# A linear-attention scan with two dense blocks on one NeuronCore: tokens taken apart by parity, the jobs of a slot in another order, and the last level's scores copied by ScalarE

## What is computed

```
for t in range(S):
    cur = einsum('bhd,bhe->bhde', u[None] * k[t], v[t])
    y[t] = einsum('bhd,bhde->bhe', r[t], state + cur)
    state = w[t][:, :, :, None] * state + einsum('bhd,bhe->bhde', k[t], v[t])
```

```
h = gelu(x @ w_in); u, v = split(h)
gated = u * (einsum('ts,bsd->btd', w_sg, layernorm(v) * g_ln) + b_sg)
x = x + gated @ w_out
xk, xr = mu * x + (1 - mu) * x_prev          # one mix for k, one for r
out = sigmoid(xr @ w_r) * ((relu(xk @ w_k) ** 2) @ w_v)
```

## Time and profile before

| | us |
|---|---|
| median of three runs | 417.6 |
| the profiled execution | 420.01 |
| its span, first to last instruction | 418.3 |
| TensorE matmuls busy | 364.8 (87%) |
| VectorE busy | 253.9 (61%) |
| ScalarE busy | 190.4 (46%) |
| GpSimd busy | 120.9 (29%) |

### The profile page before, as it was taken

How to read it: one execution, slowest core, us unless ns; L and a number is a source line. 1 busy time by engine, 2 the same in 40 slices (tenths; PEclk the granted TensorE clock), 3 DMA queues, 4 the chain that set the end, 5 groups by cost and what they waited for, 6 DMA issues and landing times.

```text
span 418.3 us, 9108 instructions
## 1 busy us (share of the span) xinstructions
PE 364.8 (87%) x3836; PEld 344.8 (82%) x3836; DVE 253.9 (61%) x384; ACT 190.4 (46%) x326; POOL 120.9 (29%) x138
## 2 busy tenths in 40 slices
PE   5665868978878698668999999999999999999997
PEld 4554657767768586568998999999999999999996
DVE  6357867687979967650655445998796311764011
ACT  4435626666774645533312416627783700565100
POOL 6705524346447343000000000610970000463000
PEclk9998958989999999969999999999999999999999
DMA  8986670606202110101000001306000011000011
GB/s 161 233 199 134 177 175 3 133 15 141 60 4 60 30 30 2 30 2 49 19 2 0 0 2 26 126 0 196 15 2 0 2 40 55 19 2 0 19 39 56
DMA packets 58584, 23.59 MB, mean 56 GB/s; under 512 B 52656, under 2 KB 56112, under 8 KB 58544
## 3 DMA queue, kind: packets, MB, share of 16 engines
q1 hardware_dynamic: 58544, 23.02, 21.8%
HBM read 18.29 MB, written 2.36 MB: 49 GB/s over the span
## 4 chain that ended last, share of the span: by engine, by line
PE 78%; issue 7%; ACT 7%; DVE 6%; DVEq 0%; ACTq 0%
PE ps L1184 20%; PE ps L1186 19%; PE ps L1185 19%; PE ps L1175 5%; PE ps L1107 5%; PE ps L1171 3%; PE ps L1140 2%; PE ps L1129 2%; ACT r L617 1%; DVE kT L860 1%; PE ps L1117 1%; ACT rU L615 1%; PE ps L1145 1%; ACT ktok L639 1%; ACT yT L672 1%
## 5 line engine op out<-in xcount | busy, mean ns | idle before, releaser
L552 POOL TENSOR_TENSOR r<-r,wb 112x768 f32<-112x768 f32 x24 | 41.3, 1732 | 83.9 <-PE ps L1175 83.9
L599 POOL TENSOR_TENSOR sq_f<-sq_f 128x384 f32<-128x384 f32 x32 | 33.8, 1071 | 74.9 <-ACT sq_f L742 74.8
L860 DVE TENSOR_TENSOR kT<-kT,wb 112x384 f32<-112x384 f32 x40 | 35.0, 876 | 18.7 <-PE ps L1175 18.5
L1027 DVE TENSOR_TENSOR ot<-ps,ee 128x384 f32<-128x384 f32 x12 | 6.7, 557 | 54.6 <-PE ps L1186 54.6
L1175 PEld LDWEIGHTS ps<-r,kT 112*64 112x64 f32 x960 | 34.3, 150 | 5.8 <-issue 3.8
L1175 PE MATMUL ps<-r,kT 112*64 112x64 f32 x960 | 38.7, 238 | 0.4 <-issue 0.2
L1012 DVE TENSOR_TENSOR sq_l<-sq_f,sq_h 128x384 fp32r<-128x384 f32 x32 | 27.7, 864 | 10.3 <-ACT sq_h L747 10.3
L1186 PE MATMUL ps<-xk_h,wk_l 128*128 128x384 f32 x96 | 32.2, 335 | 0.0
L1185 PE MATMUL ps<-xk_l,wk_h 128*128 128x384 f32 x96 | 32.2, 335 | 0.0
L1184 PE MATMUL ps<-xk_h,wk_h 128*128 128x384 f32 x96 | 32.2, 335 | 0.0
L1184 PE MATMUL ps<-wv_h,sq_h 128*128 128x384 f32 x96 | 32.1, 334 | 0.0
(11 more groups left out here) (148 smaller groups left out, 969.9 us busy)
## 6 DMA issues: line engine op xcount, KB each, us to landing
tok_w<-in_w_dram SPq DMA_DIRECT2D x16, 144.0 KB, 3.0
tok_k<-in_k_dram SPq DMA_DIRECT2D x16, 144.0 KB, 3.2
tok_r<-in_r_dram SPq DMA_DIRECT2D x16, 144.0 KB, 3.2
sgn<-in_moe_w_sg_dram SPq DMA_DIRECT2D x6, 384.0 KB, 4.7
vt<-in_v_dram SPq DMA_DIRECT2D x16, 144.0 KB, 3.3
out_dram<-ot SPq DMA_DIRECT2D x12, 192.0 KB, 1.9
xT<-yT SPq DMA_DIRECT2D x12, 144.0 KB, 2.7
win_raw<-in_moe_w_in_dram SPq DMA_DIRECT2D x1, 1536.0 KB, 8.4
```

The costliest lines, as they stand in the source:

```text
L552: nc.gpsimd.tensor_tensor(t, t, pair_of(h, 0, q).unsqueeze(1).unsqueeze(3).broadcast_to([ROWS, 2, S // (2 * h), h]), ALU.mult).then_inc(r_ ...
L599: nc.gpsimd.tensor_tensor(t, t, t, ALU.mult).then_inc(k_sq, 1)
L860: nc.vector.tensor_tensor(t, t, pair_of(h, 1, q).unsqueeze(2).broadcast_to([ROWS, S // (2 * h), h]), ALU.mult).then_inc(k_scaled, 1)
```

## The change

- The loads of `w`, `k`, `r` place even tokens in the first three of six turns and odd tokens in the last three, so even tokens come out in one PSUM bank of `turn` and odd tokens in the other. The decays `wT` stay in that order. The loads of a pair keep their sizes.
- ScalarE's six copies of r: odd first, with a semaphore of their own (`r_odd_out`), on which `first_r` now waits. k likewise: even first (`k_even_out`), and `first_k` waits on that.
- The last level: VectorE's masked copy is gone. ScalarE copies 32 x 384 elements twice (`take_last`), partitions 0 to 31 and 64 to 95, columns 32 to 63 of each block: with h = 32 the block is full.
- `ktok` is copied in one instruction over 128 partitions, not in two over 64; the zeros that kept the two chunks apart are now in `vt`, which has two planes. v is loaded with four DMAs per pair, not two, and GpSimd clears the four `vt` (1344 elements per partition each) after the masks and `r2`; `ktok` and the pads of `vt` are no longer cleared.
- `w_sg`: ScalarE rounds straight from PSUM into the high half, VectorE subtracts straight from PSUM (`low_sg`), and `turn` is free only after that. ScalarE's second pass (L792) and the six subtractions in slots 14 to 19 are gone. `w_sg` is loaded through three buffers instead of six, the last three loads later.
- Slots: level 4 before kt, r before level 3. On ScalarE the spreading of decays goes ahead of sg and k, `lay_states` follows k at once, and the last level's copy stands at the start of the odd slot. On VectorE the levels, then `low_sg` in its place, then `first_k` and `first_r` in their own slot (not the next), then `chain`.
- `gelu_u` and `high_vn` wait on y of earlier pairs instead of on levels of the last pair.

```diff
-            jobs = [("kt", a - 3), ("level", a - 2, 4), ("w", a + 1), ("level", a - 1, 2), ("sg", a - 2), ("level", a, 0),
+            jobs = [("level", a - 2, 4), ("kt", a - 3), ("w", a + 1), ("level", a - 1, 2), ("sg", a - 2), ("level", a, 0),
                     ("k", a + 1), ("u", a - 3)]
-            jobs = [("level", a - 2, 5), ("level", a - 1, 3), ("r", a + 1), ("level", a, 1), ("y", a - 3)]
+            jobs = [("level", a - 2, 5), ("r", a + 1), ("level", a - 1, 3), ("level", a, 1), ("y", a - 3)]
+    def act_jobs(slot):
+        a = slot // 2
+        if slot % 2 == 0:
+            jobs = [("kt", a - 3), ("w", a + 1), ("wm", a - 3), ("sg", a - 2), ("k", a + 1), ("sy", a - 3)]
+        else:
+            jobs = [("last", a - 2), ("r", a + 1), ("y", a - 3)]
...
-                                     src[b, 2 * p + x].rearrange("(c p) d -> p c d", p=P)
+                        sp.dma_start(tok[s][kind][:, :, 64 * x:64 * x + D].rearrange("p (two c) d -> p two c d", two=2),
+                                     src[b, 2 * p + x].rearrange("(c p two) d -> p two c d", p=P, two=2)
...
+            for s in range(4):
+                nc.gpsimd.memset(vt[s][:, :, :, :], 0.0).then_inc(late_zeroed, 1)
...
+            def take_last(q):
+                act.wait_ge(scores, level_at(q, LEVELS - 1) + 1)
+                act.wait_ge(masked, taken_at(q, LEVELS - 2))
+                for lo in (0, CH):
+                    ins = nc.scalar.copy(aT[q % 4][lo:lo + 32, :, :, 32:CH].rearrange("p c x t -> p (c x) t"),
+                                         old[lo:lo + 32, 0:HF].rearrange("p (m t) -> p m t", t=32))
+                ins.then_inc(last_taken, 1)
...
             def first_r(q):
-                dve.wait_ge(copied, turn_at[("r", q)] + 1)
+                dve.wait_ge(r_odd_out, q + 1)
...
+            def low_sg(n):
+                dve.wait_ge(copied, turn_at[("sg", n)] + 1)
+                c = slice(n * P, (n + 1) * P)
+                nc.vector.tensor_tensor(wsg_l[:, :, c].rearrange("p (b j) t -> p b j t", b=2),
+                                        turn[:, :, 0:HF].rearrange("p b (j t) -> p b j t", j=3),
+                                        wsg_h[:, :, c].bitcast(F32).rearrange("p (b j) t -> p b j t", b=2),
+                                        ALU.subtract).then_inc(sg_low, 1)
...
             def turn_free(last):
+                elif last[0] == "sg":
+                    pe.wait_ge(sg_low, last[1] + 1)
```

More of the change, by code:

```diff
@@ L63, in side_jobs @@
         return [job for job in pe_jobs(slot) if job[0] != "level"]
+    def act_jobs(slot):
[4 more added lines that the diff above has]
+            jobs = [("last", a - 2), ("r", a + 1), ("y", a - 3)]
+        jobs = [job for job in jobs if 0 <= job[1] < (C if job[0] == "sg" else NP)]
+        return jobs + EARLY_DENSE.get(slot, [])
     EARLY_DENSE = {16: [("V", 0, 0), ("V", 0, 1)], 17: [("V", 0, 2), ("V", 0, 3)], 18: [("V", 0, 4), ("V", 0, 5)],
@@ L81, in rwkv_gmlp_channel_mix_kernel @@
     for slot in range(SLOTS):
[L82 to L85, removed]
+        K_SCALES += [(q, l) for q, l in level_jobs(slot) if l] + [(q, 0) for kind, q, *_ in side_jobs(slot) if kind == "k"]
         R_SCALES += [(q, l) for q, l in level_jobs(slot) if 0 < l < DVE_R]
+        R_SCALES += [(q, 0) for kind, q, *_ in side_jobs(slot) if kind == "r"]
     POOL_SCALES = [(q, l) for q, l in LEVEL_JOBS if l >= DVE_R]
@@ L472, in _ @@
             load_pair(4)
-            for t in range(2, C):
-                load_sg(t)
+            load_sg(2)
             load_v(1)
@@ L573, in _ @@
                 nc.gpsimd.memset(wchunk[s][:, :], 0.0).then_inc(wc_zeroed, 1)
-            for z in (sy[:, :, D:CH], ktok[:, :, :, :]):
-                nc.gpsimd.memset(z, 0.0).then_inc(late_zeroed, 1)
+            nc.gpsimd.memset(sy[:, :, D:CH], 0.0).then_inc(late_zeroed, 1)
             for q, l in FIRST_JOINS:
@@ L759, in _ @@
             for slot in range(SLOTS):
-                for job in side_jobs(slot):
+                for job in act_jobs(slot):
                     if job[0] == "y":
@@ L766, in _ @@
                         gelu_u(0, job[2])
-                    elif job[0] == "u":
+                    elif job[0] == "wm":
                         spread_products(job[1])
+                    elif job[0] == "last":
+                        take_last(job[1])
+                    elif job[0] == "sy":
+                        lay_states(job[1])
                     else:
                         copy_turn(job)
-                for job in side_jobs(slot):
-                    if job[0] == "u":
-                        lay_states(job[1])
                 if slot == 0:
@@ L1032, in _ @@
             for slot in range(SLOTS):
-                for job in side_jobs(slot - 1) if slot else []:
+                for job in pe_jobs(slot):
+                    if job[0] == "level":
+                        q, l = job[1:]
+                        if l:
+                            scale_k(q, l)
+                        if 0 < l < DVE_R:
+                            scale_r(q, l)
+                        if l < LEVELS - 1:
+                            take_level(q, l)
+                    elif job[0] == "sg":
+                        low_sg(job[1])
+                for job in side_jobs(slot):
                     if job[0] == "k":
@@ L1037, in _ @@
                         first_r(job[1])
-                for q, l in level_jobs(slot):
-                    if l:
-                        scale_k(q, l)
-                    if 0 < l < DVE_R:
-                        scale_r(q, l)
-                    take_level(q, l)
+                    elif job[0] == "u":
+                        chain(job[1])
                 if slot == 0:
@@ L1046, in _ @@
                         nc.vector.memset(aT[s][:, :, :, :], 0.0).then_inc(zeroed, 1)
-                for job in side_jobs(slot):
-                    if job[0] == "u":
-                        chain(job[1])
                 for n in range(PIECES):
@@ L1163, in level_job @@
                     if l % 2:
[L1164 removed]
+                        pe.wait_ge(masked, taken_at(q, l - 1))
+                    elif q and l == 4:
+                        pe.wait_ge(last_taken, q)
                     elif q:
[L1166 removed]
+                        pe.wait_ge(masked, taken_at(q - 1, l + 1))
                 for c in range(C):
@@ L1196, in group_job @@
                 elif g < EARLY:
-                    turn_free(("r", NP - 1))
+                    turn_free([job for job in TURNS if turn_banks(job) is turn][-1])
                 if g == EARLY:
```

131 lines of the change are left out of this document (64 added, 67 removed).

## The result

The changed kernel takes 427.19 us (median of 4 runs, 423.94 to 427.66), the kernel before 418.2 us beside it (4 runs, 416.84 to 419.27). The ratio is 1.02, with a 95% interval of 1.014 to 1.026: slower, clear of noise. The forecast was 405.6 us, and its range, 398 to 413.5, does not hold the time. The profiled execution took 427.23 us, its span is 425.5.

The account below looks back on a forecast made before the run. Dense part bound by TensorE's matmuls, scan part by the order in which engines wait for each other. Terms summed to -12.0: 408.0 us against the profiled 420.0, 405.6 against the median 417.6; range 398 to 413.5.

Parts of the forecast that it names:

- the clock: Scan part: without two 2 us gaps before r the clock stays up at two places, -2.6; ends 0 and -5.7.
- turns of r: Scan part: the 7.5 us TensorE waits in five pairs for k's shared banks go, except some 0.8; -6.7.
- kt and w: Scan pairs: waits for y's copy and first_r, together 1.35 per pair, +0.5; ends -1.5 and +4.5.
- y: End of the scan part: states laid ahead of the dense activations, so the 3.0 us wait before y goes; -3.0.
- late u, first dense group: End of the scan part: shorter ktok copy starts u and first dense group earlier, -2.2; other u waits, -1.0.
- `low_sg`: VectorE's subtraction for sg straight from PSUM: 0.95 us each, the low figure, not the longest 1.84.
- The two early waits of r: Two early pairs, 3.6 us behind the copy of k: first_k's 0.55 leaves each wait; -1.1.
- k's new wait: Turn of k waits for low_sg to free turn, 0.85 at each of five places: +4.1; ends 0 and +8.6.
- The tail: End of the scan part: u and first dense group -2.2, wait before y -3.0, late u waits -1.0.
- Rival 2: Slower: sg holds the banks too long, products wait out GpSimd's, k and w wait at five places; 423.3 us, chance 0.08.
- The 4 us less that was worked out for a wait of level 3's product: Skill page's shared port: level 3's VectorE product waits out GpSimd's, gain about 4 us smaller, 409.6.
- The sentence on what would show the forecast wrong: Wrong if idle before k or w exceeds 2 us per pair, or the dense part changes over 1 us from 221.1.

Follow-up runs that it names:

- e5: Changed kernel with kt's six transposes issued 6 times for pair 0 and 4 times for pairs 1 to 3, same result; 420.34 us, 1.0027.
- e4: Changed kernel with first_r ahead of level 1's products in VectorE's queue instead of behind them; 411.06 us, 0.9831.
- e13: e4 with low_sg ahead of level 2's masked copy and VectorE's halves of w_in moved to odd slots; 406.02 us, 0.9684.
- e2: Changed kernel with level 3 ahead of the turn of r again; 429.12 us, 1.0235.
- e1: Changed kernel with kt ahead of level 4 again; 419.97 us, 1.0019.
- e11: Changed kernel with the last level's masked copy on VectorE again and ScalarE's two copies gone; 423.62 us, 1.0108.
- e16: Changed kernel with ScalarE's two last-level copies cut to 12 elements per partition, leaving out nearly all of that level's scores; 426.88 us, 1.0178.
- e3: Changed kernel with both TensorE orders put back, kt ahead of level 4 and level 3 ahead of r; 420.7 us, 1.0038.

## Why the prediction was wrong

The sum gave 408.0 for the profiled execution; it took 427.2, 19.2 more. In TensorE's own terms: the clock was to give 2.6 and took 8.4, 11.0 apart; the waits were to shrink by 9.4 and shrank by 1.2, 8.2 apart. That is the 19.2. The waits one by one (idle time of TensorE in us, by what stood behind it):

| waits ahead of | before | changed | forecast | measured |
|---|---|---|---|---|
| turns of r | 11.1 | 3.8 | -7.8 | -7.3 |
| kt and w | 17.9 | 23.4 | +0.5 | +5.4 |
| k | 0 | 0.9 | +4.1 | +0.9 |
| y | 3.0 | 0.3 | -3.0 | -2.7 |
| late u, first dense group | 10.8 | 8.7 | -3.2 | -2.1 |
| levels and sg | 2.1 | 6.1 | 0 | +4.0 |
| first loads of w and k | 5.0 | 5.7 | 0 | +0.7 |

- **kt and w: the step that failed.** It says +0.5, with `first_r` at 5.2 to 5.3 behind y and kt's end at 4.8. In the pair shown y starts at 89.09; kt ends 5.3 behind it (94.37), `first_r` 8.0 behind (97.05). So kt was 0.5 late against the step and `first_r` 2.7. The waits are 1.20 + 2.79 = 4.0 us in this pair, where the step has 1.35; in the whole kernel they grew by 5.4. The step took "no more of it than is in the time before": it kept the collisions at the level where it had seen them, level 5, though moving level 4 on TensorE also moves GpSimd's product of level 4, onto level 1. Even its upper end, +4.5 with 1.0 per pair, was for another product, and too small. Of the 13.1 us that the kernel before idled ahead of w, its largest group of waits, the step looked at 0.48 only, and not at the early pair where this very collision stood (51.61 above). Of the 2.7 us, the two stretched products are 2.0: 2.27 less 0.95, and 1.19 less the 0.55 or so of one alone.
- **The clock.** The two waits it looked at (before r) did go. The term priced what their going gives, and its bad end was 0, since nothing else was to make the clock fall. The first of its two places paid: the pair that had 0.76 works 2.4 us less. But behind the new waits at w it falls in every pair, and in the tail, where it was to stay up, TensorE works 6.4 us longer. e5 puts 6.9 us on it.
- **Turns of r, y, `ktok`, `low_sg`: right.** Of the 7.5 before r 0.6 are left, for 0.8 forecast; before y 0.3 of 3.0; 6.22 of the 6.93 stay, for 6.2 forecast; `low_sg` takes 0.956, for 0.95. The two early waits of r shrank by 0.4 only (3.6 to 3.2), where 1.1 was forecast.
- **The levels: at nothing without a reason.** The sum has no wait for them. At 35.62 level 4 waits 1.46 us for GpSimd's product of r, at 52.11 1.56 for VectorE's product of k; with the smaller ones it is 4.0 more than before.
- **k's new wait: too high** (+4.1). With w held up, k does not come to a closed door; it idles 0.9 in all. In e4 and e13, without w's wait, it is there (1.53 above).
- **The tail.** The waits of y, of the late u jobs and of the first dense group shrank by 4.8 us, where 6.2 was forecast, and the clock took 6.4, so that the gain is gone.
- **The rivals.** Rival 2 had the sign and the mechanism, products of VectorE that wait out GpSimd's, and 423.3 us, at a chance of 0.08. It placed them at level 4 or 2 and `low_sg`, in front of k above all (w had 1.7 of it), and without the clock. So its time came near for a reason that was half right. The 4 us less that was worked out for a wait of level 3's product shows in no run: with level 3 ahead of r again (e2) the kernel is no faster. The sentence on what would show the forecast wrong, an idle time of over 2 us per pair before w, is what happened.

**The chain, as shown.** Level 4 ahead of kt brings GpSimd's product from 2.85 us behind the start of VectorE's (e1) to 0.38 ahead of it (7.2 us); without VectorE's masked copy level 4 and GpSimd's product behind it come sooner still, and first (e11: 3.6; e16: not ScalarE's copies); `first_r` is last in that queue, and w behind it (e4: 16.1 for its place alone); the waits lower the clock (e5: 6.9). These overlap and don't add up.

**Open.** Why the kernel before loses 2.5 us by level 4's place without a longer product of r. What holds e3 at 420.7 with both orders back, at a clock of 0.931: the longer wait for the copy of y before kt is seen there, but no run with both orders back takes away what delays that copy. Why the clock falls more often in the tail. And how the 16 us of e4 divide between the collision and the clock, since no kernel had the one without the other over all pairs.

## What to carry to other kernels

When jobs of one engine change places, list the work that each releases on the others, with its new start, and look what it now meets. Find the last instruction in the queue on which the busiest engine's next job depends, and put it as early as its inputs allow: here one call, moved ahead of products that nobody needed yet, turned a loss of 2% into a gain of 1.7%, and 3.2% with its followers. A wait of 2 to 3 us in each period is priced with what it does to the clock, not by its length alone. And rank the waits of the kernel before by size first: of the largest group here, 13.1 us ahead of w, the forecast looked at 0.5.

## What the hardware did that I had not expected

- A shift of 0.6 us between two starts decides who pays. With GpSimd first by 0.38, VectorE's product takes 2.27 for 0.95; with VectorE first by 0.21, GpSimd's takes 2.12 for the 1.52 of e1. The later one waits until the other is through.
- Less work made the kernel slower: without the 0.57 us copy on VectorE it takes 3.6 us more (the changed kernel against e11), and ScalarE's copies in its place are not the reason (e16).
- Waits of 1.20 and 2.79 us, with the 0.79 us of kt between them, were enough to put the granted clock at the lower level for the four jobs behind them, in each pair. In e1 w ran at it too, behind a wait of 1.90 before kt and 0.17 of its own. In e13 single waits of 1.36 and 1.53 us left it at 1.00.
- Useless transposes paid: 84 more matmuls, and 6.9 us less.
